# An attention and feed-forward kernel: where the first weights and operands of the feed-forward are made while attention still runs

## The reference, cut to what matters

```python
scores = scale * np.matmul(q, k.transpose(0, 1, 3, 2))
mask = (rel >= 0) & (rel < window)                        # window 128
scores = np.where(mask, scores + bias[None], -1000000000.0)
attn = np.exp(scores - max); attn = attn / (sum + 1e-09)
x = np.matmul(attn, v) -> (2304, 512)
h = x @ w_in;  x = (h / (1 + exp(-1.702 h))) @ w_out       # layer 1
h = x @ w_in2; x = clipped_square(h) @ w_out2              # layer 2
```

## Time and profile before

| | us |
|---|---|
| median of 3 runs | 882.63 |
| lowest and highest | 881.43, 884.73 |
| the profiled execution | 883.84 |
| span in its profile | 882.1 |
| granted clock of TensorE, mean | 0.988 of full speed |

### The profile page before, as it was taken

How to read it: one execution, slowest core, us unless ns; L and a number is a source line. 1 busy time by engine, 2 the same in 40 slices (tenths; PEclk the granted TensorE clock), 3 DMA queues, 4 the chain that set the end, 5 groups by cost and what they waited for, 6 DMA issues and landing times.

```text
span 882.1 us, 15505 instructions
## 1 busy us (share of the span) xinstructions
PE 859.3 (97%) x5746; PEld 852.8 (97%) x5746; DVE 710.4 (81%) x985; ACT 536.6 (61%) x788; POOL 113.5 (13%) x78
## 2 busy tenths in 40 slices
PE   7998889999999999999999999999999999999998
PEld 7998879999999999999999999999999999999998
DVE  6886788457798877677997987988989779889794
ACT  4875667566675565667754546676556576765431
POOL 3788487300000000000000000000000000000000
PEclk9999898999999999999999999999999999999999
DMA  8998692168766553677857465388554653788822
GB/s 204 241 259 227 174 249 81 42 262 283 281 237 213 203 212 129 244 257 278 315 204 282 160 223 179 146 305 304 211 203 169 237 192 141 273 288 293 310 81 72
DMA packets 63369, 191.17 MB, mean 217 GB/s; under 512 B 7488, under 2 KB 14400, under 8 KB 59456
## 3 DMA queue, kind: packets, MB, share of 16 engines
q1 hardware_dynamic: 63296, 190.18, 64.5%
HBM read 117.81 MB, written 72.35 MB: 216 GB/s over the span
## 4 chain that ended last, share of the span: by engine, by line
PE 86%; DVE 5%; POOL 4%; issue 2%; SPq 1%; ACT 1%; DMA 1%; DVEq 0%; POOLq 0%; ACTq 0%
PE ps L1041 79%; PE ps L1009 3%; PE ps L975 2%; POOL qk_hi L888 2%; PE ps L988 2%; POOL k_lo L884 1%; DVE wst L1572 1%; DVE probs L1540 1%; DVE qk_hi L1516 1%; DMA qk_raw<-qkT 1%; POOL w_first L908 1%; PE ps L1018 1%; SPq L568 1%; DVE heads_out L1553 1%; PE ps L1003 0%
## 5 line engine op out<-in xcount | busy, mean ns | idle before, releaser
L1041 PE MATMUL ps<-arena,w_first 128*128 128x384 f32 x1764 | 331.6, 336 | 0.9 <-ACT ps L1288 0.8
L1041 PEld LDWEIGHTS ps<-arena,w_first 128*128 128x128 f32 x1764 | 310.8, 188 | 2.4 <-issue 1.7
L1041 PE MATMUL ps<-arena,w_rest 128*128 128x384 f32 x1260 | 240.8, 337 | 0.9 <-ACT ps L1288 0.8
L1041 PEld LDWEIGHTS ps<-arena,w_rest 128*128 128x128 f32 x1260 | 220.1, 188 | 2.0 <-issue 1.7
L1645 DVE TENSOR_TENSOR arena<-raw_first,arena 128x768 fp32r<-128x768 f32 (+1 forms) x114 | 148.9, 1319 | 77.8 <-ACT arena L1260 77.8
L1260 ACT ACTIVATE arena<-raw_first 128x768 fp32r<-128x768 f32 (+1 forms) x120 | 132.0, 1117 | 45.6 <-DVE raw_first L1604 39.3
L1041 PE MATMUL ps<-w_rest,arena 128*128 128x256 f32 x945 | 132.5, 281 | 0.0
L1041 PEld LDWEIGHTS ps<-w_rest,arena 128*128 128x128 f32 x945 | 121.1, 189 | 0.1
L1041 PE MATMUL ps<-w_first,arena 128*128 128x256 f32 x567 | 88.0, 282 | 0.0
L1645 DVE TENSOR_TENSOR arena<-raw_rest,arena 128x1536 fp32r<-128x1536 f32 (+1 forms) x48 | 71.4, 1487 | 11.3 <-ACT arena L1260 11.2
L1041 PEld LDWEIGHTS ps<-w_first,arena 128*128 128x128 f32 x567 | 76.0, 189 | 0.0
(11 more groups left out here) (115 smaller groups left out, 975.0 us busy)
## 6 DMA issues: line engine op xcount, KB each, us to landing
gd<-g SPq DMA_DIRECT2D x24, 1536.0 KB, 6.1
raw_rest<-gd SPq DMA_DIRECT2D x32, 768.0 KB, 5.7
qk_raw<-qkT SPq DMA_DIRECT2D x60, 288.0 KB, 6.9
wst<-w_pairs SPq DMA_DIRECT2D x32, 512.0 KB, 6.5
raw_first<-gd SPq DMA_DIRECT2D x16, 768.0 KB, 6.1
yd<-ust SPq DMA_DIRECT2D x6, 1536.0 KB, 6.3
wd<-ust SPq DMA_DIRECT2D x4, 1536.0 KB, 9.3
raw_first<-yd SPq DMA_DIRECT2D x4, 1536.0 KB, 7.0
```

The source lines that it names most:

```text
L1041: last = nc.tensor.matmul(to, stationary, moving, start=start and n == 0, stop=n == len(steps) - 1, skip_group_check=True)
```

## The change

On POOL: the three sums of weight pair 0 go from behind heads 11, 12, 13 to one behind head 11 and two behind head 13; its first split goes behind head 15, its second behind head 17, and its third to VectorE (step 41). POOL also takes two splits of weight pair 1, behind heads 23 and 25. The operand splits go from behind heads 25, 26, 28, 29 to behind 21, 27, 29, 31.

On VectorE: the sums of weight pair 1 go from step 43 to steps 46 (one) and 51 (two); it keeps only one split of that pair, in step 71; S1 and S2 go from steps 58 and 63 to 61 and 66; the sums of weight pair 2 go from step 66 to step 76 (one) and behind the last scores (two). ScalarE's roundings follow, those of weight pair 2 behind step 79. SP issues the load of weight pair 3 later, behind the store of pair 11.

```diff
--- before.py
+++ after.py
@@ -761,10 +761,10 @@
                 load_weights(2)
             if q == 12:
                 load_first_x(1)
-            if q == 14:
-                load_weights(3)
         for q in range(PAIR_COUNT - X_STORE_LAG, PAIR_COUNT):
             store_pair(q)
+            if q == PAIR_COUNT - X_STORE_LAG:
+                load_weights(3)
 
         def up_transfers(u):
             load_x(u, 1)
@@ -928,12 +928,17 @@
         split_rest_keys()
         for head in range(2, 2 * PAIR_COUNT):
             split_head(head)
-            if head in (11, 12, 13):
-                add_weights(0, head - 11)
-            if head in (14, 15, 16):
-                split_weights(0, head - 14)
-            if head in (25, 26, 28, 29):
-                split_operand((A11, S1, S2, A12)[(25, 26, 28, 29).index(head)])
+            if head == 11:
+                add_weights(0, 0)
+            if head == 13:
+                add_weights(0, 1)
+                add_weights(0, 2)
+            if head in (15, 17):
+                split_weights(0, (15, 17).index(head))
+            if head in (23, 25):
+                split_weights(1, (23, 25).index(head))
+            if head in (21, 27, 29, 31):
+                split_operand((A11, S1, S2, A12)[(21, 27, 29, 31).index(head)])
         sum_s3()
         sum_s4()
         split_operand(S3)
@@ -1272,10 +1277,14 @@
                 make_bias((3, 6, 11).index(m) + 1)
             if (q := pair_at(m, COPY_LAG)) is not None:
                 copy_pair(q)
-            if m in (30, 45, 70):
-                round_both((30, 45, 70).index(m))
-            if m in (55, 59, 64, 65, 77, 79):
-                round_operand(0, (55, 59, 64, 65, 77, 79).index(m))
+            if m in (30, 46):
+                round_weights((30, 46).index(m), 0)
+            if m in (32, 53):
+                round_weights((32, 53).index(m), 1)
+            if m in (44, 62, 67, 69, 77, 79):
+                round_operand(0, (44, 62, 67, 69, 77, 79).index(m))
+            if m == ALL_STEPS:
+                round_both(2)
 
         def seed_b(D, n):
 
@@ -1561,11 +1570,12 @@
                 last = nc.vector.tensor_copy(x_pairs[rows, pair, 4 * P:SEQ], xt_bank[rows, rows])
             last.then_inc(pair_tail_copied, 1)
 
-        def add_weights(w):
-
-            w_staged(dve, w)
-            dve.wait_ge(w_ready, 3 * nth(w))
-            for step in range(3):
+        def add_weights(w, steps=(0, 1, 2)):
+
+            if 0 in steps:
+                w_staged(dve, w)
+                dve.wait_ge(w_ready, 3 * nth(w))
+            for step in steps:
                 if step:
                     dve.wait_ge(w_added, 3 * nth(w) + step)
                 to, a, b = w_sum(w, step)
@@ -1578,15 +1588,12 @@
             dve.wait_ge(w_rounded, 2 * nth(w) + 2)
             nc.vector.tensor_tensor(rest[:, :, 1], w_others(w), f32(rest[:, :, 0]), ALU.subtract).then_inc(w_ready, 2)
 
-        def split_weights_part(w, step):
-
-            dve.wait_ge(w_rounded, 2 * nth(w) + (1 if step == 0 else 2))
-            if step == 0:
-                to, a, hi = made_first(w)[:, 1], w_b11(w), made_first(w)[:, 0]
-            else:
-                some = slice(3 * step - 3, 3 * step)
-                to, a, hi = made_rest(w)[:, some, 1], w_others(w)[:, some], made_rest(w)[:, some, 0]
-            nc.vector.tensor_tensor(to, a, f32(hi), ALU.subtract).then_inc(w_ready, 1)
+        def split_last_weights(w):
+
+            dve.wait_ge(w_rounded, 2 * nth(w) + 2)
+            dve.wait_ge(w_ready, 3 * nth(w) + 2)
+            nc.vector.tensor_tensor(made_rest(w)[:, 3:6, 1], w_others(w)[:, 3:6], f32(made_rest(w)[:, 3:6, 0]),
+                                    ALU.subtract).then_inc(w_ready, 1)
 
         def sum_operand(k, i):
             if i == S1:
@@ -1625,14 +1632,14 @@
                 split_rest()
             if m in (1, 2):
                 round_head(m + 1)
-            if m == 43:
-                add_weights(1)
-            if m in (46, 48, 51):
-                split_weights_part(1, (46, 48, 51).index(m))
-            if m in (58, 63):
-                sum_operand(0, S1 if m == 58 else S2)
-            if m == 66:
-                add_weights(2)
+            if m in (41, 71):
+                split_last_weights(0 if m == 41 else 1)
+            if m in (46, 51):
+                add_weights(1, (0,) if m == 46 else (1, 2))
+            if m in (61, 66):
+                sum_operand(0, S1 if m == 61 else S2)
+            if m in (76, ALL_STEPS):
+                add_weights(2, (0,) if m == 76 else (1, 2))
             for head in range(SPLIT_RING, 2 * PAIR_COUNT):
                 if m == last_use(head - SPLIT_RING) + (1 if head == SPLIT_RING else CAST_LAG[head % 2]):
                     round_head(head)
```

## The result

The changed kernel takes 873.61 us (median of 4 runs, 873.14 to 875.48) where the kernel before takes 883.13 (4 runs); the ratio is 0.9896, with a 95% interval of 0.9872 to 0.9921. Measured once more beside other kernels it was 0.9911 (0.9896 to 0.9927), 874.32 us. The forecast was 868.7: 14 us less, of which 9.5 came. The profiled execution took 873.14 us, with a span of 871.4; the profile of the second measurement has a span of 873.8. One execution among all that follow, of the run with odd heads on ScalarE and the loads moved, took 3387.62 us at a granted clock of 0.24, and is left out.

The account below looks back on a forecast made before the run. TensorE paces attention; the feed-forward only starts earlier. Ten stretches, 80.9 + 3 VectorE + 0.5 POOL + 3.7 SP = 88.1 against 102.2: 14.1 less, 13.9 with 0.2 at the end; median 868.7 us, own range 865.5 to 873.5.

Parts of the forecast that it names:

- the wide one: Whole kernel: the wider forecast range, 861.5 to 876 us, which takes in R2 but for its edge.
- R2: Rival, chance 0.17: loads of heads 20 to 23 all late, two or three half-clock waits; gain 6 to 9, 873.5 to 876.5.
- What bounds: Feed-forward matmuls hold 79% of the span unchanged; in attention TensorE sets the pace, 8.09 us per undisturbed pair.
- The waits that go: Attention: TensorE's waits of 2.62 us for POOL and 2.39, 1.48, 3.16 for VectorE's write-outs vanish with their half clock.
- The lump of sums: VectorE's three sums at once, 2.97 us, right ahead of a write-out, made TensorE wait 2.39 us, half clock after.
- the sign of being wrong on VectorE: TensorE waiting over 1 us for write-outs behind steps 61 or 66 would refute the VectorE term.
- The SP term: SP stands still 6 us before loading weight pair 2; head 20 comes 3.1 us late; cost 3.7 us, bounds 0 and 7.
- The VectorE and POOL terms: Attention: VectorE's seven separate pieces cost 3 us (0 to 4.5); POOL's splits stretched beside VectorE cost 0.5 (0 to 2).
- VectorE's room: Undisturbed pair in attention: VectorE is busy 7.31 of 8.09 us, leaving 0.78 us to spare.

## Why the prediction was partly right

*The time:* 873.61 us is 0.1 above the forecast's own range (865.5 to 873.5), and in the wide one by the room that R2 gave it. The measured gain is two thirds of the forecast one.

*What bounds, and that only the start of the feed-forward moves:* right, 719.6 and 719.8 us behind it.

*The waits that go:* right for POOL's, which comes back at its old size (2.64 us, with half clock) when that part is undone. Half right for the write-outs. The lump of sums does make TensorE wait, as its return shows (5.25 us, with half clock). But waits for write-outs did not go: four are left (1.58, 0.97, 1.58 and 1.54 us), with two half-clock spells, where 2.39, 1.48 and 3.16 were to vanish. One of them, at 122.12, stands behind step 61, which the prediction had named as the sign of being wrong on VectorE.

*The SP term, 3.7 us:* the mechanism was right, to 1.2 us in its time (79.7 said, 80.89 seen), the size too large: the wait was 1.27, and no half-clock spell followed it. The load was there when forecast (87.5 for 87.6), but VectorE, late itself, came to it at 86.23 and not at 84.5. The same kind of hold three pairs later, worth 1.51, was overlooked, so that the sum over loads is 3.0 in the profiled execution. What of it is on the path is less: taking the waits away gave 1.6 between the profiles.

*The VectorE and POOL terms, 3 + 0.5 us:* this is the step that failed. They measured 8.1 or more, outside the bounds of both together (4.5 and 2). The prediction took VectorE's room (0.78 us a pair) and POOL's (8.09 less 7.8) one at a time, and so found that a piece on each would nearly fit. In the trace they take turns, so their pieces add up: 9.5 us a pair. The sign was in the earlier trace rows and in the earlier trace rows: a rounding of 0.76 and one of 1.56, a split of 1.79. The prediction read these as a higher price for some instructions, up to 4.5 us, and not as a sum that fills the pair. The price that it did not count is on the roundings: those of heads 8 to 31 took 27.9 us before and 33.7 after, though nothing about them was changed. The rule of the Trainium skill that POOL and VectorE contend when VectorE has two SBUF inputs (GPSIMD Engine Reference, Specifications) pointed the right way. The trace agrees for the two-input subtractions (2.10 and 1.76 us for 768 columns where 0.95 is the time alone), and the roundings, which have one input, took turns as well. What the runs show is that the two take turns; how much of the 8.1 that makes in each pair is a sum over rows, and no run takes the turns away alone.

*The rivals:* R2's number came true (873.5 to 876.5), by luck and not by its mechanism: of heads 20 to 23 only head 20 came late, and the one spell that can be compared in the first profile cost nothing.

## What to carry to other kernels

Before work is spread over two engines, add up what each holds of what they share: here, the time of VectorE's and POOL's SBUF-to-SBUF instructions together has to stay under the pace of a pair, and not each engine's alone. That is needed and not enough: VectorE's own instructions with their waits for turns have to fit too (9.18 of 9.29 us in the run with the operand splits on VectorE). Work on the critical engine should not stand ahead of what the matrix engine waits for: of the two parts that were undone, this one was worth more, 2 to 3 us. Ahead of every wait that is made later, look at what the same queue issues behind it.

## What the runs showed of the hardware that was not expected

- VectorE's rounding (fp32, 128x1152) and its subtractions of two SBUF tensors took turns with POOL's subtractions in the traces of both kernels. VectorE's ended 0.60 to 0.68 us (rounding) or 0.81 to 0.83 (one of 768 columns) after the POOL instruction that they met, whatever POOL's length (0.74 to 1.83 us), and POOL's were longer by what VectorE took meanwhile (2.02 for 1.41).
- ScalarE's rounding of the same 1152 columns took 1.15 to 1.16 us in all sixteen cases of the two runs that brought it in, with POOL at work throughout in six of them and idle in three.
- The clock of TensorE fell to 1.2 GHz some 1.6 us after the end of a wait of 1.58 us, in two pairs, and did not after waits of 1.54 and 0.97 in others of the same execution. In the second profile it fell after waits of 1.58 and 1.53 us and not after 1.56 and 1.51.
